# A fused attention, token-mixing and gated-MLP kernel on one core: last chunk's z in two parts, its theta inside a token unit, own banks for the last channel tiles, and a ring of eight banks in the second block

## What is computed

```python
# 1. linear attention with decay, 8 heads of 48
state = alpha_t[:, None] * state + outer(k_t, v_t);  x_t = q_t @ state
# 2. first block (384 channels)
theta = x @ w_theta
zr, zi = x * cos(theta), x * sin(theta)
y = w_tok_r @ zr + w_tok_i @ zi            # over the 768 tokens
u = x + y
x2 = u + relu(u @ w_ch)
# 3. second block (1024 = 512 + 512 hidden channels)
h = relu(x2 @ w_in);  u, v = h[:, :512], h[:, 512:]
v_n = (v - mean(v)) / sqrt(var(v) + 1e-6)
out = (u * (w_spatial @ v_n + b_spatial)) @ w_out
```

## Time and profile before

| | us |
|---|---|
| median of 3 runs | 626.73 (626.13 to 627.73) |
| the profiled execution, its own time | 626.28 |
| its span, first to last instruction | 624.6 |
| PE busy with matmuls | 591.7 (95%) |
| DVE, POOL, ACT busy | 363.1, 257.7, 224.0 |
| mean granted PE clock, share of full | 0.986 |

### The profile page before, as it was taken

One profiled execution on the slowest core, in us unless ns is written; L12 is line 12 of the kernel. 1 busy time (PEld: TensorE's weight loads), 2 busy tenths in 40 slices (PEclk: granted clock), 3 DMA queues, 4 the chain that ended last, 5 costly groups with the idle time before them and its releaser, 6 DMA issues.

```text
span 624.6 us, 11166 instructions
## 1 busy us (share of the span) xinstructions
PE 591.7 (95%) x4608; PEld 560.6 (90%) x4608; DVE 363.1 (58%) x565; ACT 224.0 (36%) x410; POOL 257.7 (41%) x205
## 2 busy tenths in 40 slices
PE   4778989999999999999997999999999999999998
PEld 3667889999999999999996978998999899989997
DVE  5788666787786776877734037846333633373132
ACT  2544556343343444433434114623131313131210
POOL 5475578353463353644513017245313531352130
PEclk9978999999999999999998999999999999999999
DMA  8551321132141231320323073010220020002002
GB/s 314 203 178 65 111 82 64 64 102 66 65 165 65 61 106 65 105 95 32 102 102 114 0 266 114 8 70 2 76 77 2 0 77 1 0 1 77 0 2 77
DMA packets 20259, 49.54 MB, mean 79 GB/s; under 512 B 1648, under 2 KB 15216, under 8 KB 19696
## 3 DMA queue, kind: packets, MB, share of 16 engines
q1 hardware_dynamic: 20208, 48.81, 22.8%
HBM read 39.37 MB, written 9.44 MB: 78 GB/s over the span
## 4 chain that ended last, share of the span: by engine, by line
PE 86%; DVE 5%; ACT 3%; POOL 3%; issue 2%; DMA 0%; DVEq 0%; ACTq 0%; POOLq 0%
PE psY L409 22%; PE psF L508 8%; PE psS L508 8%; PE psC L391 7%; PE psC L428 7%; PE psS L486 5%; PE psS L342 5%; PE psF L476 5%; PE psF L486 3%; PE psS L496 3%; PE psF L496 3%; PE psF L370 3%; PE psS L476 3%; PE psF L375 2%; PE psF L332 2%
## 5 line engine op out<-in xcount | busy, mean ns | idle before, releaser
L948 POOL TENSOR_TENSOR z_lo<-cos_sin,z_hi 128x768 fp32r<-128x768 f32 x24 | 44.0, 1833 | 125.6 <-ACT z_hi L598 125.6
L1012 POOL TENSOR_TENSOR gated_lo<-u_gated,gated_hi 128x384 fp32r<-128x384 f32 x32 | 32.4, 1013 | 125.4 <-ACT gated_hi L698 125.3
L409 PE MATMUL psY<-tok_r_hi,z_hi 128*128 128x384 f32 x144 | 52.5, 365 | 4.7 <-POOL z_lo L948 4.3
L747 DVE TENSOR_TENSOR_SCAN akq<-akq,rtotal 128x516 f32<-128x516 f32 x24 | 54.7, 2281 | 0.7
L409 PE MATMUL psY<-tok_r_hi,z_lo 128*128 128x384 f32 x144 | 48.5, 337 | 0.0
L409 PE MATMUL psY<-tok_r_lo,z_hi 128*128 128x384 f32 x144 | 48.5, 337 | 0.0
L409 PE MATMUL psY<-tok_i_lo,z_hi 128*128 128x384 f32 x144 | 48.4, 336 | 0.0
L409 PE MATMUL psY<-tok_i_hi,z_lo 128*128 128x384 f32 x144 | 48.4, 336 | 0.0
L409 PE MATMUL psY<-tok_i_hi,z_hi 128*128 128x384 f32 x144 | 48.4, 336 | 0.0
L931 POOL TENSOR_TENSOR akq<-akq,after 128x512 f32<-128x512 f32 x24 | 44.7, 1862 | 4.9 <-DVE after L738 4.9
L698 ACT ACTIVATE gated_hi<-u_gated 128x384 fp32r<-128x384 f32 x32 | 16.8, 526 | 81.0 <-DVE u_gated L886 81.0
(11 more groups left out here) (141 smaller groups left out, 1747.3 us busy)
## 6 DMA issues: line engine op xcount, KB each, us to landing
akq<-akq SPq DMA_DIRECT2D x23, 770.0 KB, 4.5
v<-v_in SPq DMA_DIRECT2D x24, 192.0 KB, 4.7
x_dram<-u_f SPq DMA_DIRECT2D x8, 576.0 KB, 3.7
x_raw<-x_dram SPq DMA_DIRECT2D x4, 1152.0 KB, 5.5
out<-ot SPq DMA_DIRECT2D x24, 192.0 KB, 1.9
raw_tok_r<-w_tok_rT SPq DMA_DIRECT2D x6, 384.0 KB, 7.8
raw_tok_i<-w_tok_iT SPq DMA_DIRECT2D x6, 384.0 KB, 8.7
raw_sp<-w_spT SPq DMA_DIRECT2D x1, 2304.0 KB, 8.9
```

The costliest lines, as they stand in the source:

```text
L409: mm = pe.matmul(psY[:, j, 0:HALF], Z[s][l][:, q, tile(j)], W[m][:, s, half(h)], start=(s == 0 and q == 0 and n == 0), stop=(s == CHUNKS - ...
L747: dve.tensor_tensor_scan(ALPHA[s], ALPHA[s], rtotal[:, 1:], rtotal[:, 0:1], ALU.mult, ALU.add).then_inc(decayed, 1)
L948: pool.tensor_tensor(Z[c][1][:], trigs[g % 2][:], f(Z[c][0][:]), ALU.subtract).then_inc(z_lo, 1)
```

## The change

What it does:
- `RING` goes from 4 to 8: the ring of the second block also takes the three psY banks and psC.
- Channel tiles 21, 22 and 23 get the banks psC, psY[2] and psY[1]; only a tile in psC waits for `x2_made` of the one before. `values(0, 4)` and `values(0, 5)` wait for the last u and the last x2, whose banks they reuse.
- For chunk 23 alone the unit behind transpose_x is cut in two: channel tile j = 0, then `angles(23)`, then j = 1 and 2.
- In DVE's order of every chunk `make_x2` now stands ahead of `xT_low`.
- For chunk 23 multiply_z, z_high and z_low are each cut in two instructions of 128x384, first q = 1 (sine), then q = 0 (cosine), and the unit (6,5) is `token_mix_last`: nine matmuls of q = 1, which wait for the first z_lo, then nine of q = 0.
- DVE's `make_u` of half 6 stands ahead of the three `in_lo`.
- The wait for all six `sp_lo` ahead of the first spatial_mix becomes a wait for one of them at each step s of the first spatial_mix of a batch.

```diff
-RING = 4
+RING = 8
...
-                 psF[:, 0], psF[:, 1]]
+                 psF[:, 0], psF[:, 1], *[psY[:, j] for j in range(CT)], psC[:]]
+
+        last_banks = (banks[7], banks[6], banks[5])
...
-            sp.wait_ge(z_mul, ALL)
+            sp.wait_ge(z_mul, ALL + 1)
...
-            def token_mix(unit):
+            def token_mix(unit, tiles=range(CT)):
...
-                if s < CHUNKS - 1:
+                if s < CHUNKS - 1 and CT - 1 in tiles:
                     mm.then_inc(mixed, 1)
 
-            def channel_mix(n, angles_before):
+            def token_mix_last():
+
+                k, s = HALVES * (BATCH - 1), CHUNKS - 1
+                for q in (1, 0):
+                    pe.wait_ge(z_lo, ALL + 1 - q)
+                    for j in range(CT):
+                        for n, (l, m) in enumerate(PASSES):
+                            mm = pe.matmul(psY[:, j, 0:HALF], Z[s][l][:, q, tile(j)], (WR, WI)[q][m][:, s, half(0)],
+                                           start=False, stop=(q == 0 and n == 2))
+                        if q == 0:
+                            mm.then_inc(y_made, 1)
+
+            def channel_mix(n, angles_before, bank=psC):
...
-                need(pe, x2_made, n)
+                if bank is psC:
+                    need(pe, x2_made, n)
...
-                    token_mix(yb)
-                    angles(g, 0 if n is None else n + 1)
+                    if g == ALL - 1:
+                        token_mix(yb, (0,))
+                        angles(g, n + 1)
+                        token_mix(yb, (1, 2))
+                    else:
+                        token_mix(yb)
+                        angles(g, 0 if n is None else n + 1)
...
                     if i == 0:
                         pe.wait_ge(vn_lo, b * CHUNKS + s + 1)
+                        pe.wait_ge(sp_lo, s + 1)
...
-                token_mix(yb)
+                if c:
+                    token_mix(yb)
+                else:
+                    token_mix_last()
             pe.wait_ge(in_lo, CT)
             values(0, 0)
             values(0, 1)
             for m in range(CT):
-                channel_mix((HALVES * b + 1) * CT + m, ALL)
+                channel_mix((HALVES * b + 1) * CT + m, ALL, last_banks[m])
             for i in range(2, CHUNKS):
+                if i == 4:
+                    pe.wait_ge(u_made, BATCH * TILES)
+                if i == 5:
+                    pe.wait_ge(x2_made, BATCH * TILES)
                 values(0, i)
...
-                if b == 0:
-                    pe.wait_ge(sp_lo, CHUNKS)
...
             sines(ALL - 1)
-            z_high(ALL - 1)
+            act.wait_ge(y_made, HALVES * (BATCH - 1) * CT)
+            for n, q in enumerate((1, 0)):
+                act.wait_ge(z_mul, ALL + n)
+                act.activation(Z[CHUNKS - 1][0][:, q], trigs[(ALL - 1) % 2][:, q], ACT.Copy).then_inc(z_hi, 1)
             act.wait_ge(in_in, 16)
-            act.wait_ge(z_lo, ALL)
+            act.wait_ge(z_lo, ALL + 1)
...
+                    make_x2(tile_of(b, c))
                     xT_low(g)
-                    make_x2(tile_of(b, c))
                     update_state(g)
...
             reduce_angle(ALL - 1)
-            multiply_z(ALL - 1)
+            for n, q in enumerate((1, 0)):
+                last = (ALL - 1) % 2
+                dve.wait_ge(trig, 3 * ALL - 2 + 2 * n)
+                dve.tensor_tensor(trigs[last][:, q], x[last][:], trigs[last][:, q], ALU.mult).then_inc(z_mul, 1)
             make_x2(tile_of(b, 0))
+            make_u(HALVES * b)
             for j in range(CT):
                 dve.wait_ge(in_hi, j + 1)
                 dve.tensor_tensor(WN[1][:, j, :], raw_in[:, j, :], f(WN[0][:, j, :]), ALU.subtract).then_inc(in_lo, 1)
-            make_u(HALVES * b)
...
-                make_x2((HALVES * b + 1) * CT + m)
+                make_x2((HALVES * b + 1) * CT + m, last_banks[m])
...
-            z_low(ALL - 1)
+            for n, q in enumerate((1, 0)):
+                pool.wait_ge(z_hi, ALL + n)
+                pool.tensor_tensor(Z[CHUNKS - 1][1][:, q], trigs[(ALL - 1) % 2][:, q], f(Z[CHUNKS - 1][0][:, q]),
+                                   ALU.subtract).then_inc(z_lo, 1)
```

More of the change, by code:

```diff
@@ L403, in token_mix @@
                     pe.wait_ge(z_lo, k // HALVES * CHUNKS + s + 1)
-                for j in range(CT):
+                for j in tiles:
                     if s == 0:
@@ L427, in channel_mix @@
                     for k, (l, m) in enumerate(PASSES):
-                        mm = pe.matmul(psC[:, 0:HALF], WC[l][:, j, tile(m_out)], U[m][:, j, :],
+                        mm = pe.matmul(bank[:, 0:HALF], WC[l][:, j, tile(m_out)], U[m][:, j, :],
                                        start=(j == 0 and k == 0), stop=(j == CT - 1 and k == 2))
@@ L808, in make_u, with make_x2 @@
                     dve.tensor_tensor(UF[h][:, m], psY[:, m, 0:HALF], XK[k % 3][:, m], ALU.add).then_inc(u_made, 1)
-            def make_x2(n):
+            def make_x2(n, bank=psC):
                 if n is None:
@@ L814, in make_x2 @@
                 dve.wait_ge(ch_made, n + 1)
-                dve.scalar_tensor_tensor(out=UF[h][:, m], in0=psC[:, 0:HALF], scalar=0.0, in1=UF[h][:, m],
+                dve.scalar_tensor_tensor(out=UF[h][:, m], in0=bank[:, 0:HALF], scalar=0.0, in1=UF[h][:, m],
                                          op0=ALU.max, op1=ALU.add).then_inc(x2_made, 1)
```

## The result

| | before | after |
|---|---|---|
| median of the runs, us | 626.43 (4 runs, 625.32 to 627.73) | 621.92 (4 runs, 620.63 to 622.20) |
| profiled execution, us | 626.28 | 620.63 |
| its span, us | 624.6 | 618.9 |

The ratio of after to before is 0.9923, with a 95% interval of 0.9899 to 0.9947. (The median before has one run more than the 626.73 that the forecast started from.) That is 4.5 us less where 6.0 were forecast: inside the range, and within 0.2 us of the rival in which the clock falls once more (622.1).

A forecast was written before the change was run, and what follows sets the result against it. PE, busy 95% of the span, was taken as the bound, so only its losses could be won. 3.4 us (tile 18 earlier) + 2.6 us (sp_lo step by step) = 6.0; 626.73 - 6.0 = 620.7 us, range 618.6 to 622.8.

The forecast's parts named there:

- the clock falls once more: Rival (0.25): PE's 2.1 us wait ahead of tile 18 lowers the clock, slow matmuls cost 1.4 us; 622.1 us.
- Part 1: Chunk 23: theta starts after the unit's first channel tile; theta and the chain behind it come 1.65 us earlier.
- Part 2: Chunk 23: z made in halves, both ready before PE asks; the 3.3 us wait and the slow stretch go.
- Part 3: u of half 6: u_lo on POOL meets in_lo on DVE; tile 18 starts 3.4 us earlier, bounds 5.1 and 2.1.
- By turns: POOL's u_lo and DVE's in_lo alternate, one after the other; the last u_lo ends at 339.05, tile 18 starts at 339.1.
- Part 4: Tiles 21 to 23 and ring: gaps (1.9 us) and bank wait (1.4) go, but neither shortens the end.
- Part 5: First spatial_mix: sp_lo awaited step by step leaves three matmuls behind the last sp_lo; 2.6 us won.
- no meeting at the port: Rival (0.18): in_lo slips behind the u_lo or only one turn is lost; 7.7 us less, 619.0 us.
- in_lo goes first: Rival (0.1): in_lo precedes u_lo or DVE keeps its turn; 4.7 us less, 622.0, or 623.4 with the clock's fall.
- the lead is not used: Rival (0.03): PE comes late to spatial_mix or its short waits slow it; 3.4 us alone, 623.3 us.
- slower: Rival (0.02): DVE's new order makes PE wait for xT_lo in the loop, 17 chunks losing 0.47 us each; 628.7 us.

The follow-up runs named there:

- e1: Changed kernel with DVE's three in_lo moved behind make_x2 of tile 18, away from the u_lo of half 6; 619.02 us, ratio 0.9879 to the kernel before.
- e2: Changed kernel with 11 matmuls of no use filling PE's wait for u_lo ahead of tile 18; 620.07 us, ratio 0.9904 to the kernel before.
- e7: Kernel before with only the ring of eight, own banks for tiles 22 and 23, and sp_lo awaited step by step; 624.10 us, ratio 0.9961.
- e3: Changed kernel with SP loading the bias ahead of raw_sp and raw_out; 619.47 us, ratio 0.9889 to the kernel before.
- e4: Changed kernel with the one wait for all six sp_lo ahead of the first spatial_mix put back; 626.33 us, ratio 0.9995 to the kernel before.
- e8: Changed kernel with the ring of the second block back at four banks (RING = 4 alone); 624.99 us, ratio 0.9967 to the kernel before.
- e9: Changed kernel with make_u of half 6 back behind the three in_lo on DVE; 622.81 us, ratio 0.9936 to the kernel before.
- e5: Changed kernel with both in_lo behind make_x2 of tile 18 and the bias loaded first; 616.32 us, ratio 0.9833 to the kernel before.

## Why the prediction was right, and where it was wrong

The direction, the range and nearly all terms held. What was wrong is the branch that I took as the likeliest: the sum put the clock at nothing.

- **Part 1, theta inside the unit: right.** PE idled for 0.3 us and theta began with xT_lo (320.86 against 320.82). Relative to xT_hi of chunk 23 it starts at 1.13 us instead of 2.93, so 1.8 earlier; with the restart 1.65 were forecast.
- **Part 2, z in halves: right.** Two z_lo in 1.98 us, no wait of PE, no slow stretch there.
- **Part 3, the port: right.** "By turns" put the end of the last u_lo 4.7 us behind the first one's start, and it was 4.90. The three u_lo of this group averaged 1.6 us, the three in_lo 1.93. PE waited 2.1 us, as written. e1 shows the cause: without the meeting both take their old time. That DVE and POOL hold each other up is shown; what they share, no run here tells. Tile 18 starts at 337.88 - 319.73 = 18.15 behind xT_hi instead of 342.48 - 321.10 = 21.38: 3.2 us earlier, 3.4 forecast.
- **The clock: wrong.** The sum has no term for it; I gave it a quarter of the chance as a rival and costed it at 1.4. The wait of 2.1 us did make the clock fall in the changed kernel, and e2, which differs in nothing but PE's work in that wait, has the clock at full. It cost 1.5 to 1.6: of the 3.2 us that tile 18 had won, the last sp_lo keeps 1.7 (73.4 behind xT_hi, 396.20 - 321.10 = 75.1 before). The trace of before had shown the fall behind a gap of 2.0 us, closer to 2.1 than the 1.4 us without one, so by the rule of the nearest row the rival should have been the forecast: 620.7 + 1.4 = 622.1, and 621.92 was measured. The Trainium skill ("TensorE: Matmul & The Clock Gate", section "HAM oscillation — how this bites in real kernels") warns of idle gaps of PE too, but the gaps that it means are longer than this one, so by it alone the forecast would have stood. Here 2.1 us of wait were followed by 0.50 of the clock, and the measurement decides.
- **Part 4, gaps and bank wait off the path: right.** e7's longer wait of DVE for the bias shows where the 1.9 us went, and e3 gives 2.0 of it back by one reordered load.
- **Part 5, 2.6 us: right in its place, incomplete in its worth.** The end is 4.3 earlier and the last sp_lo 1.7, which leaves 2.6. With its banks and ring alone (e7) it gives 2.5. In the changed kernel its absence costs 5.4 (e4), since the wait it takes apart would have been 4.5 us long and would have brought the clock down.
- **The rivals:** "no meeting at the port", "in_lo goes first" (u_lo at 332.93, in_lo at 333.12), "the lead is not used" and "slower" did not happen. For the last, the distance between the kernels' chunks stays 1.37 to 1.38 from chunk 4 to chunk 17, so DVE's new order costs the loop nothing.

## What to carry to other kernels

Price a wait of PE by its length and by the clock behind it: here 2.1 us of idle cost another 1.5, and 4.5 us another 3, and matmuls of no use in the gap of 2.1 us gave the 1.5 back. When a step is moved ahead of another on DVE, look at what POOL does in that moment: moving make_u ahead won at most 0.3 us as made, and 3.4 came when in_lo was moved out of the way as well. And when a gain vanishes, find the load that the next chain starts on; a small load queued behind 3 MB of others was worth 2 us.

## What the hardware showed that I had not expected

- The time from the bias' issue to its landing was not steady when it was queued behind raw_sp and raw_out: 9.9 to 12.1 us over nine traces, with the same order on SP's queue. It is the group of loads that varies: raw_sp took 8.8 to 9.0 us in seven of them, and there the bias landed 11.8 to 12.1 us after raw_sp was issued; in e8 and e9 raw_sp took 9.7 and 10.5, and it was 12.8 and 13.6. Loaded first the bias took 4.6 (e3) and 4.0 (e5).
- The 4 runs of e3 spread over 1.4 us and the 4 of e5 over 1.1, the 10 of e8 and of e7 over 3.3 and 4.3. How much of that is the loads, the clock or only the number of runs is open. The clock has a part: of e7's runs the fastest (620.95) has a mean granted clock of 0.989, the other nine 0.984 or 0.986.
- The fall of the clock may not come in every run. By the windows above one fall takes some 1.7 us of full clock, which I estimate as 0.003 of the mean. All four runs of the changed kernel have 0.986, and e1 and e5, without the wait, 0.989. But two of the four runs of e3 and two of the six of e9, which have the wait, have 0.989 as well. Only the profiled runs show where the clock fell, so this is a hint and not shown. It would make e3's median, 2.45 us under the changed kernel's, better than its stretch.
- Behind the wait of 2.1 us the clock fell after PE had resumed: at 338 to 339 in the changed kernel, with PE at work since 337.88. In longer waits it fell before PE resumed: in e4 at 393.9 in a wait that ended at 394.92, after which it stayed low up to 400.8, and in the kernel before in the window 333 to 334 (0.64), ahead of the matmul at 333.74.
- With instructions queued on both engines, DVE and POOL took turns through all three pairs. The single lengths of in_lo and u_lo in the changed kernel (ns min/median/max) show it: every in_lo, also the shortest, waited. The first u_lo of the group took 1.01 us, and the two behind it nearly twice that, 1.99 and 1.97.

```profile
L987 POOL TENSOR_TENSOR u_lo<-u_f,u_hi x24: 1002/1014/1991, 94.6 to 363.1; 128x384 fp32r<-128x384 f32 x24
...
L927 DVE TENSOR_TENSOR in_lo<-raw_in,in_hi x3: 1911/2006/2031, 333.1 to 336.9; 128x1024 fp32r<-128x1024 f32 x3
```
